# A new order of work for the steady batches of a fused attention and mixture kernel

## The reference, cut to what matters

```
# 1: windowed attention, 8 heads of 64: q k^T masked to 32 keys (plain, heads 0-3; every 4th key, heads 4-7)
x = attention(q, k, v)                                   # (4, 576, 512)
# 2: per batch, 4 experts e of full causal attention, head size 64
q, k, v = x @ wq[e], x @ wk[e], x @ wv[e]
a = softmax(causal(q @ k.T / 8));  ye = a @ v @ wo[e]
x2 += gate[e] * ye                                       # gate: top 2 of 4 by x @ w_gate, softmax
# 3: each token goes to one of 8 experts (argmax of logits, or the expert of the token before)
out[b, s] = p[e] * (relu(x2 @ w1[e]) @ w2[e])
```

## Time and profile before

| what | us |
|---|---|
| median of three runs (730.52 to 733.12) | 730.98 |
| the profiled execution | 725.44 |
| its span, first to last instruction | 723.6 |
| PE busy (98% of the span) | 707.6 |
| PE weight loads busy (72%) | 524.0 |
| DVE busy (42%) | 306.9 |
| ACT busy (40%) | 287.5 |

### The profile page before, as it was taken

One profiled execution on the slowest core, in us unless ns is written; L12 is line 12 of the kernel. 1 busy time (PEld: TensorE's weight loads), 2 busy tenths in 40 slices (PEclk: granted clock), 3 DMA queues, 4 the chain that ended last, 5 costly groups with the idle time before them and its releaser, 6 DMA issues.

```text
span 723.6 us, 15576 instructions
## 1 busy us (share of the span) xinstructions
PE 707.6 (98%) x5265; PEld 524.0 (72%) x5266; DVE 306.9 (42%) x928; ACT 287.5 (40%) x852; POOL 98.5 (14%) x145
## 2 busy tenths in 40 slices
PE   8999989999999999999999999999999999999997
PEld 7887866777667876777665777777777777777774
DVE  3762788437882588714656412111211121112111
ACT  2671578426883368723530222321232123212320
POOL 4300001000010000100003112111211121112113
PEclk9999999999999999999999999999999999999999
DMA  8385225421282122300017107440250771001101
GB/s 173 92 198 137 67 58 149 126 55 34 59 218 74 38 48 68 133 23 1 18 42 262 52 30 258 150 154 29 81 224 29 261 264 43 29 29 37 43 29 37
DMA packets 86515, 69.69 MB, mean 96 GB/s; under 512 B 69118, under 2 KB 69150, under 8 KB 86464
## 3 DMA queue, kind: packets, MB, share of 16 engines
q1 hardware_dynamic: 78816, 44.73, 22.2%
q0 software_dynamic: 7648, 24.29, 10.3%
HBM read 118.12 MB, written 11.27 MB: 179 GB/s over the span
## 4 chain that ended last, share of the span: by engine, by line
PE 92%; DVE 3%; ACT 2%; issue 1%; POOL 1%; DMA 1%; POOLq 0%; DVEq 0%; ACTq 0%
PE bank L1206 22%; PE bank L1217 21%; PE bank L778 9%; PE bank L774 5%; PE bank L869 5%; PE bank L700 4%; PE bank L828 4%; PE bank L857 4%; PE bank L740 3%; PE bank L799 3%; PE bank L683 3%; PE bank L713 2%; PE bank L676 2%; PE bank L1189 1%; PE bank L804 1%
## 5 line engine op out<-in xcount | busy, mean ns | idle before, releaser
L1206 PEld LDWEIGHTS bank<-pt,stage_b 128*128 128x128 f32 x1344 | 155.0, 192 | 10.0 <-issue 10.0
L1217 PE MATMUL bank<-w_all,raw_all 128*128 x352 | 158.2, 593 | 0.0
L1206 PE MATMUL bank<-pt,stage_b 128*128 128x128 f32 x1344 | 156.9, 275 | 0.0
L1627 ACT ACTIVATE raw_all<-bank 128x512 f32<-128x512 f32 x44 | 26.3, 597 | 215.9 <-PE bank L1206 215.9
L1217 PEld LDWEIGHTS bank<-w_all,raw_all 128*128 128x128 f32 x352 | 63.6, 191 | 63.6 <-issue 63.6
L2172 DVE TENSOR_SCALAR raw_all<-bank,p_slot 128x512 f32 x21 | 15.8, 750 | 208.9 <-PE bank L1217 208.9
L617 POOL DMA_INDIRECT out_dram<-raw_all,idx_out x25 | 37.6, 1506 | 246.7 <-DVE raw_all L2172 229.8
L778 PE MATMUL bank<-stage_b,w_all 128*128 128x288 f32 x256 | 70.0, 421 | 0.1
L1396 ACT ACTIVATE pr<-sm,negmax_a 96x80 f32<-96x80 f32 (+1 forms) x168 | 59.6, 358 | 3.1 <-DVE negmax_a L1677 2.9
L778 PEld LDWEIGHTS bank<-stage_b,w_all 128*128 128x128 f32 x256 | 47.5, 194 | 14.7 <-issue 3.3
L1385 ACT COPY w_sb<-bank 128x256 f32<-128x256 f32 (+5 forms) x93 | 38.2, 420 | 31.4 <-PE bank L828 29.9
(11 more groups left out here) (226 smaller groups left out, 921.1 us busy)
## 6 DMA issues: line engine op xcount, KB each, us to landing
w_sb<-in_moe_w_dram SPq DMA_DIRECT2D x19, 2048.0 KB
w_all<-in_moe_w_dram SPq DMA_DIRECT2D x19, 2048.0 KB
w_sb<-in_moe_w_dram POOLq DMA_DIRECT2D x12, 512.0 KB, 5.2
w_all<-in_moe_w_dram POOLq DMA_DIRECT2D x12, 512.0 KB, 5.5
raw_all<-in_q_dram SPq DMA_DIRECT2D x32, 144.0 KB
raw_all<-in_k_dram SPq DMA_DIRECT2D x32, 144.0 KB
mixture_rows<-y_sb SPq DMA_DIRECT2D x16, 256.0 KB, 2.6
v_dil<-in_v_dram SPq DMA_DIRECT2D x42, 80.0 KB, 3.2
```

What stands on the lines that cost most here:

```text
L1206: last = pe.matmul(ps[half][:, f * P:(f + 1) * P], w1_sb[:, 0, c * F + at:c * F + at + P] if buf is None else w1_fix[:, c, at:at + P], xT[ ...
L1217: last = pe.matmul(ps[5], hidT[:, half * HALF + n * P:half * HALF + (n + 1) * P], w2_sb[:, bass.ds(buf, 1), half, n * D:(n + 1) * D].rearr ...
```

## The change

The pieces of the steady periods take the order that `pe_last` has: values at n = 4 to 8, second halves of q and k at n = 9 to 12. The latter go to bank X, where `pe_use` also works, each placed among the groups of stage 1 and the first units of stage 2. `x_free` gets a count `late` of such pieces to wait for. The lists of the first period keep their text under new names (`pe_first`, `act_first`, `dve_first`); the steady periods get new lists (`pe_steady`, `act_steady`, `dve_steady`) with the same calls in another order. In the routing, three counts of the matmuls into unused banks change.

```diff
         def proj_piece(m, n):
-            if m == B - 1 and 4 <= n < 4 + NT:
+            if 4 <= n < 4 + NT:
                 return "v", n - 4, 0
-            if m == B - 1 and n >= 4 + NT:
+            if n >= 4 + NT:
                 n -= NT
-            if n < 8:
-                return ("q", "k")[n % 2], (n // 2) % 2, n // 4
-            return "v", n - 8, 0
+            return ("q", "k")[n % 2], (n // 2) % 2, n // 4
...
-        def x_free(pe, m, a, use, ys):
+        def x_free(pe, m, a, use, ys, late=0):
...
+                if late > 0:
+                    pe.wait_ge(proj_moved[1], m * NPROJ_B[1] + 4 + (late + 1) // 2)
+                    pe.wait_ge(proj_moved[0], m * NPROJ_B[0] + 5 + late // 2)
...
         def proj_bank(m, n):
-            if m == B - 1 and n >= 4 + NT:
-                return (SA, PA)[(n - 4 - NT) % 2]
-            return S2[n % 2] if n < (4 if m == B - 1 else 8) else (PT, O2)[n % 2]
+            if n >= 4 + NT:
+                return (SA, PA)[(n - 4 - NT) % 2] if m == B - 1 else X
+            return S2[n % 2] if n < 4 else (PT, O2)[n % 2]
...
+            elif n >= 4 + NT and m < B - 1:
+                x_free(pe, m, a, use, ys, n - 4 - NT)
...
+        def pe_steady(pe, m, a):
+            pe_use(pe, m, a, 0, 0, 0)
+            pe_project(pe, m, 3)
+            pe_use(pe, m, a, 1, 0, 0)
+            pe_project(pe, m, 4)
+            pe_use(pe, m, a, 2, 0, 0)
+            pe_scores2(pe, m, 0)
+            pe_use(pe, m, a, 3, 0, 0)
+            pe_project(pe, m, 5)
+            pe_use(pe, m, a, 4, 0, 0)
+            pe_scores(pe, a, 0)
+            pe_use(pe, m, a, 5, 0, 0)
+            pe_project(pe, m, 6)
+            pe_use(pe, m, a, 6, 0, 0)
+            pe_scores(pe, a, 1)
+            pe_project(pe, m, 7)
+            pe_use(pe, m, a, 7, 0, 0)
+            pe_scores(pe, a, 2)
+            pe_use(pe, m, a, 8, 0, 0)
+            pe_project(pe, m, 8)
+            pe_use(pe, m, a, 9, 0, 0)
+            pe_scores(pe, a, 3)
+            pe_probs(pe, a, 0)
+            pe_project(pe, m, 9, a, 10, 0)
+            pe_scores(pe, a, 4)
+            pe_scores2(pe, m, 1)
+            pe_use(pe, m, a, 10, 0, 1)
+            pe_values(pe, a, 0)
+            pe_probs(pe, a, 1)
+            pe_project(pe, m, 10, a, 11, 0)
+            pe_probs(pe, a, 2)
+            pe_probs2(pe, m, 0, 0)
+            pe_scores(pe, a, 5)
+            pe_use(pe, m, a, 11, 0, 2)
+            pe_values(pe, a, 1)
+            pe_probs2(pe, m, 0, 1)
+            pe_scores2(pe, m, 2)
+            pe_project(pe, m, 11, a, 12, 0)
+            pe_scores(pe, a, 6)
+            pe_probs2(pe, m, 1, 0)
+            pe_scores2(pe, m, 3)
+            pe_probs2(pe, m, 1, 1)
+            pe_values2(pe, m, 0)
+            pe_project(pe, m, 12, a, 12, 0)
+            pe_probs2(pe, m, 2, 0)
...
+            pe_out(pe, m, a, 4, 16, 4)
+            pe_project(pe, a, 2)
+            pe_logits(pe, m, a, 3)
+            pe_logits(pe, m, a, 4)
...
-            turn_wide(5)
+            turn_wide(6)
...
-            turn_wide(3, 0)
+            turn_wide(2, 0)
...
-            turn_wide(2, 0)
+            turn_over(pe, ps[0], 5)
             turn_x(0, True)
...
+        def dve_steady(dve, m, a):
+            move_use_d(dve, a, 0)
+            move_use_d(dve, a, 1)
+            move_use_d(dve, a, 2)
+            move_proj(dve_copy, dve, m, 4)
...
+            dve_mask(dve, a, 3)
+            dve_gates(dve, m, 2)
+            dve_gates(dve, m, 3)
+            move_use_d(dve, a, 10)
...
+            dve_mask(dve, a, 8)
+            dve_norm(dve, a, 5)
+            dve_sums2(dve, m, 4)
+            dve_norm2(dve, m, 4, 0)
+            move_use_d(dve, a, 13)
```

More of the change, by code:

```diff
@@ L658, in x_free, with pe_use @@
                         pe.wait_ge(y_moved[i], n)
-        def pe_use(pe, m, a, n, ys):
+                if late > 0:
+                    pe.wait_ge(proj_moved[1], m * NPROJ_B[1] + 4 + (late + 1) // 2)
+                    pe.wait_ge(proj_moved[0], m * NPROJ_B[0] + 5 + late // 2)
+        def pe_use(pe, m, a, n, ys, late=0):
             if a is None:
@@ L664, in pe_use @@
             s = i % 2
-            x_free(pe, m, a, n, ys)
+            x_free(pe, m, a, n, ys, late)
             if j == 0:
@@ L760, in pe_project @@
                     pe.wait_ge(masked2, m * SUBS)
-            first_v = 4 if m == B - 1 else 8
-            if n == first_v:
+            if n == 4:
                 pe.wait_ge(wor_m, 4)
@@ L788, in pe_scores2 @@
                 for half in range(2):
-                    pe.wait_ge(proj_moved[half], m * NPROJ_B[half] + (2 if m == B - 1 else 4))
+                    pe.wait_ge(proj_moved[half], m * NPROJ_B[half] + 2)
             else:
                 pe.wait_ge(masked2, m * SUBS + sub(w, 0))
-            if m == B - 1 and w in (4, 5):
+            if w in (4, 5):
                 pe.wait_ge(proj_moved[1], m * NPROJ_B[1] + w + 1)
@@ L859, in pe_values2, with pe_out @@
             last.then_inc(o2_done, 1)
-        def pe_out(pe, m, a, t, use):
+        def pe_out(pe, m, a, t, use, late=4):
             if m is None:
@@ L866, in pe_out @@
                 pe.wait_ge(o2_moved[p], m * NT + t + 1)
-            x_free(pe, m, a, use, t)
+            x_free(pe, m, a, use, t, late if a is not None else 0)
             for p in range(PAIR_E):
@@ L1042, in pe_period @@
             pe_project(pe, a, 2)
+        def pe_steady(pe, m, a):
[43 more added lines that the diff above has]
+            pe_probs2(pe, m, 2, 0)
+            pe_values2(pe, m, 1)
+            pe_scores(pe, a, 7)
+            pe_probs2(pe, m, 2, 1)
+            pe_use(pe, m, a, 12, 0, 4)
+            pe_scores2(pe, m, 4)
+            pe_probs(pe, a, 3)
+            pe_scores(pe, a, 8)
+            pe_probs2(pe, m, 3, 0)
+            pe_values(pe, a, 2)
+            pe_values2(pe, m, 2)
+            pe_probs(pe, a, 4)
+            pe_probs2(pe, m, 3, 1)
+            pe_use(pe, m, a, 13, 0, 4)
+            pe_values(pe, a, 3)
+            pe_scores2(pe, m, 5)
+            pe_values(pe, a, 4)
+            pe_probs(pe, a, 5)
+            pe_probs2(pe, m, 4, 0)
+            pe_use(pe, m, a, 14, 0, 4)
+            pe_scores(pe, a, 9)
+            pe_values2(pe, m, 3)
+            pe_use(pe, m, a, 15, 0, 4)
+            pe_scores2(pe, m, 6)
+            pe_probs(pe, a, 6)
+            pe_probs2(pe, m, 4, 1)
+            pe_scores(pe, a, 10)
+            pe_values(pe, a, 5)
+            pe_out(pe, m, a, 0, 16, 4)
+            pe_probs(pe, a, 7)
+            pe_scores(pe, a, 11)
+            pe_logits(pe, m, a, 0, 6)
+            pe_values(pe, a, 6)
+            pe_probs2(pe, m, 5, 0)
+            pe_values2(pe, m, 4)
+            pe_probs2(pe, m, 5, 1)
+            pe_probs(pe, a, 8)
+            pe_scores(pe, a, 12)
+            pe_values(pe, a, 7)
+            pe_scores2(pe, m, 7)
+            pe_probs(pe, a, 9)
+            pe_values2(pe, m, 5)
+            pe_probs2(pe, m, 6, 0)
+            pe_scores2(pe, m, 8)
+            pe_probs2(pe, m, 6, 1)
+            pe_values(pe, a, 8)
+            pe_out(pe, m, a, 1, 16, 4)
+            pe_probs(pe, a, 10)
+            pe_logits(pe, m, a, 1, 9)
+            pe_values(pe, a, 9)
+            pe_probs2(pe, m, 7, 0)
+            pe_scores2(pe, m, 9)
+            pe_values2(pe, m, 6)
+            pe_probs2(pe, m, 7, 1)
+            pe_scores(pe, a, 13)
+            pe_values(pe, a, 10)
+            pe_probs(pe, a, 11)
+            pe_probs2(pe, m, 8, 0)
+            pe_values2(pe, m, 7)
+            pe_values(pe, a, 11)
+            pe_probs(pe, a, 12)
+            pe_probs2(pe, m, 8, 1)
+            pe_out(pe, m, a, 2, 16, 4)
+            pe_probs(pe, a, 13)
+            pe_logits(pe, m, a, 2, 12)
+            pe_values(pe, a, 12)
+            pe_values2(pe, m, 8)
+            pe_values(pe, a, 13)
+            pe_probs2(pe, m, 9, 0)
+            pe_out(pe, m, a, 3, 16, 4)
+            pe_probs2(pe, m, 9, 1)
+            pe_project(pe, a, 0)
+            pe_values2(pe, m, 9)
+            pe_project(pe, a, 1)
+            pe_out(pe, m, a, 4, 16, 4)
+            pe_project(pe, a, 2)
+            pe_logits(pe, m, a, 3)
+            pe_logits(pe, m, a, 4)
@@ L1877, in dve_period @@
             move_x(dve_copy, dve, m, a, 12)
+            move_out2(dve_copy, dve, m, 9)
+            move_proj(dve_copy, dve, a, 0)
+            dve_logits(dve, m)
+            move_proj(dve_copy, dve, a, 2)
+        def dve_steady(dve, m, a):
[3 more added lines that the diff above has]
+            move_proj(dve_copy, dve, m, 4)
+            move_use_d(dve, a, 4)
+            dve_mask(dve, a, 0)
+            dve_mask2(dve, m, 0, 0)
+            move_use_d(dve, a, 5)
+            dve_mask2(dve, m, 0, 1)
+            move_use_d(dve, a, 6)
+            dve_mask(dve, a, 1)
+            dve_norm(dve, a, 0)
+            move_proj(dve_copy, dve, m, 6)
+            dve_mask(dve, a, 2)
+            move_use_d(dve, a, 8)
+            dve_norm(dve, a, 1)
```

(89 more changed lines are left out.)

131 lines of the change are left out of this document (116 added, 15 removed).

## The result

The changed kernel takes **719.37 us** (718.71 to 721.39, four executions) against 731.05 for the kernel before: ratio 0.984, interval 0.981 to 0.987. That is 11.7 us less; I had forecast 5.3, with a range down to 720.5. The profiled executions differ by 5.8 us only (725.44 and 719.62). Almost the whole miss lies in what I took as constant between them: the distance from the profiled execution to the median. Ratios and their intervals leave out executions more than 1.5% above the fastest of their kernel; medians and ranges count them.

What follows compares the result with a forecast made beforehand. The prediction took PE, busy for 98% of the span, as the bound. Fewer waits in three steady periods (4.5 us) and routing (0.8 us) took 5.3 us off 730.98, giving 725.7 us, range 720.5 to 731.

Steps and rivals of the forecast that it cites:

- A period loses 3.3 us by its waits, in 11.6 us: Steady period before: PE's waits for DVE and ACT copies, read from start to start, cost 3.3 us.
- New waits of 1.8 us, a period of 84.2: Steady periods, new order: hand count of 2.0 us of waits, taken as 1.8; period 84.2 us, 1.5 less.
- floor of 82.4: Steady period: the 82.4 us it would take without any waits on PE.
- the term of 4.5 us: Steady periods: 1.5 us less in each, 4.5 us over three.
- The wait at `pe_use(3)`: Steady period, bank X: two uses must be 1.27 us apart with 0.67 between; a sure new wait of 0.6 us.
- Routing 0.8: Routing: changed counts of wide and short calls bring 0.15 us before a product and 0.65 before slot 0's transposes.
- Nearly all waits go (722.1): Rival, steady periods: only the 0.6 us at `pe_use(3)` stays; gain 8.9 us, 722.1 us; chance 0.27.
- Load of pair 2: Rival, SP's load waiting for `pe_use(3)`: 8.4 us instead of 6.1 makes it late; around 728 to 730; chance 0.05.
- Bank X binds: Rival, steady periods: eight hand-overs of the single bank cost 4.8 us against 3.3 saved; 734.7 us; chance 0.10.
- The median of the runs shown stood 5.5 us above that execution, and I carry this over: Whole kernel: the 5.5 us from profiled execution to median stay the same after the change.
- The profiled execution would take 720.1: Whole kernel: 5.3 us off the profiled 725.44 us gives 720.1 us.

Runs made afterwards that it cites:

- e11: Changed kernel with one ACT copy (unit 3's first transposes) moved ahead of the exponential of unit 4: 718.5 to 720.9 us, median 719.73.
- e5: Kernel before with two short matmul calls into bank O2 at each of four waits of a steady period: 723.76 to 726.15 us, median 724.32.
- e4: Kernel before with one wide routing call more (6 instead of 5) ahead of the product that waits for DVE: 723.5 to 739.5 us, median 732.5.
- e12: Changed kernel with eight dummy DVE copies and eight short matmul calls filling PE's wait in each steady period: 726.4 to 727.5 us, median 727.07.
- e6: Changed kernel with eight chained dummy DVE copies in each steady period, so that PE stands some 2 us: 729.5 to 737.3 us, median 733.0.
- e9: Kernel before with short matmul calls filling only the waits behind pe_use 11 and 12: 731.4 to 739.9 us in six executions.
- e1: Kernel before, unedited, run again: twelve executions, 723.9 to 750.5 us.
- e3: Kernel before with only the three routing counts changed (6 wide, 2 wide, 5 short): 723.3 to 738.9 us, median 731.0.

## Why the prediction was right and wrong, point by point

- **A period loses 3.3 us by its waits, in 11.6 us.** The crowd is there, and the change dissolved it. Idle time shows 2.0 of the 3.3; the rest is my reading from start to start.
- **New waits of 1.8 us, a period of 84.2.** 84.7 measured, so 2.3 us by the same floor of 82.4: the term of 4.5 us was 3.2. The three waits that show come to some 1.3 of the 2.3 from start to start; whether the other 1.0 is short hand-overs or a floor put too low, the traces don't separate. The first unit's transposes come 24.7 us into the period (24.6 forecast), its scores at 4.7 (4.5). The wait at `pe_use(3)` is there and sure, at 1.18 and not 1.27 us. Of the smaller ones, `pe_project(10)` and `pe_probs2(4, 0)` lose 0.1 and not 0.3 and 0.4; in their place are 0.3 at `pe_use(10)`, behind ACT's copy of a projection, and 0.5 at the transposes of unit 3, where ACT's copy stands behind an exponential (e11 moves it, and the wait is gone). The count was good, its places half so.
- **Routing 0.8.** 0.9 measured: nothing up to the first product, as forecast, then 0.30 where I had 0.15 and at most 0.2, and 0.61 where I had 0.65.
- **Nearly all waits go (722.1).** This rival's number is the nearest to 719.4, but not its mechanism: it leaves one wait of 0.6 us, and the work gained 4.0 us and not 8.9.
- **Load of pair 2.** It is issued 6.0 us into the period (5.8 forecast), and PE waits for no load.
- **Bank X binds.** It does not: its two waits come to 0.7 us a period from start to start. The Trainium skill (PSUM — Partial Sum Buffer, Summary: rules for kernel authors) has matmuls go to a different bank than the one that is being read. What a single bank costs, the trace shows: the next write comes 1.18 us behind a k's transposes, and other work fills most of that.
- **The median of the runs shown stood 5.5 us above that execution, and I carry this over.** This is the step that failed. The forecast carries 5.5 us unchanged from before to after; after the change the median stands 0.3 us below the profiled execution, so 5.8 of the 6.3 us that I missed lie here. The offset was no constant of measuring. It was time at half clock, most of it behind the crowd of waits that the change dissolves, and the profiled execution had none of it in its steady periods. I had the signs: a median outside what the profile explained, and a clock of 0.996 in a kernel bound by PE. I counted each wait at its own length in every case of the forecast; e5, which keeps the periods as long as they were and takes 7.5 us off, shows that this was wrong.
- **The profiled execution would take 720.1.** It took 719.62, but by luck. The work gave 4.0 us and not 5.3. The other 1.7 are the half clock at 56.1 us, in the first period, which the change leaves alone; none of the other thirteen profiles has it. In all, the 11.7 us are 4.0 of work and some 7.7 of clock, where I had 5.3 and nothing.

What stays open: why the same waits bring on the half clock in one period and not in the next of one execution (e4), and how few are still too many. Filled, the half clock of the steady periods is gone (e5, e12); put back, it comes (e6). That idle time alone is what counts is not shown. A filling is also work, and the new order also stands four projections of 2 us among the short products; no run tells the one from the other. That the clock also fell behind 92.10 us without idle time (e4), and that e9 fell behind 0.69 us of it, argues that the kind of work around the waits matters.

## What to carry to other kernels

Where PE is the bound, price a wait twice: by its length, and by the clock behind it. Before forecasting from one profile, compare its time and granted clock with the timed runs; timed runs that lie above it at lower clocks say that the profile lacks a cost which the change may remove or add. A crowd of short waits can be filled with matmuls into a free bank, which tests the cause in one run and here took 7.5 us off the median, where the change took 11.7.

## What the runs showed of the hardware

In the crowd of waits of the kernel before, PE never stood longer than 0.47 us at a time, some 2 us in 11.6, and the clock still fell to half, for 13.7 us (e1) or 17.1 us (e3, e4, e9), in some periods and executions and not in others. A stretch of 17.1 us cost 7.2 us (e9). Waits of 2.1 us (e6) brought stretches of 3.4 to 6.8 us. The clock also fell behind 92.10 us in which PE had no idle time, for 3.4 us (e4). The Trainium skill (TensorE: Matmul & The Clock Gate, A second HAM failure mode: psum-queue depth-cycling) tells of short idle times between groups of matmuls that make the clock swing between its two levels; the traces agree for the steady periods (clock 0.50 at 272.30 in e1, behind idle times of 0.2 to 0.5 us).
